# Attention, a routed mixture of experts and an MLP on one core: scores by quarters of the array, and a batch's keys side by side

## What is computed

```python
def _attn_ref(q, k, v, n_sink, window):          # q, k, v: 4 x 8 x 768 x 64, n_sink 4, window 128
    scores = scale * np.matmul(q, k.transpose(0, 1, 3, 2))
    pos = np.arange(S)
    is_sink = pos[None, :] < int(n_sink)
    rel = pos[:, None] - pos[None, :]
    in_window = (rel >= 0) & (rel < int(window))
    keep = is_sink | in_window
    scores = np.where(keep, scores, -1000000000.0)
    scores = scores - np.max(scores, axis=-1, keepdims=True)
    a = np.exp(scores)
    a = a / (np.sum(a, axis=-1, keepdims=True) + 1e-09)
    return np.matmul(a, v).astype(np.float32)
...
    x = np.ascontiguousarray(attn_out.transpose(0, 2, 1, 3)).reshape(B * S, H * D)   # 3072 x 512
    x = _moe_ref(x=x, **moe_kwargs)      # top 1 of 8 experts, 512 -> 1024 -> 512, relu, times the gate
    return _moe2_ref(x=x, **moe2_kwargs) # (h - tanh(h)) @ w_out with h = x @ w_in, 512 -> 2048 -> 512
```

## Time and profile before

| | us |
|---|---|
| runs of the kernel before, median of 3 | 1074.44 (1074.23 to 1078.64) |
| the profiled execution | 1071.83 |
| its span | 1070.1 |
| PE busy over the span | 1058.0 (99%) |
| DVE, ACT, POOL busy | 651.6, 474.8, 504.2 |

### The profile page before, as it was taken

The page is one execution under the profiler, slowest core; times in us unless marked ns, Lnnn a source line. Parts: engine busy times, 40 slices in busy tenths (PEclk is TensorE's granted clock), DMA queues, the critical chain, the costliest instruction groups (busy, mean ns, idle before and its releaser), DMA issues.

```text
span 1070.1 us, 17027 instructions
## 1 busy us (share of the span) xinstructions
PE 1058.0 (99%) x5919; PEld 866.1 (81%) x5919; DVE 651.6 (61%) x1393; ACT 474.8 (44%) x1013; POOL 504.2 (47%) x522
## 2 busy tenths in 40 slices
PE   9999999999999999999999999999999999999997
PEld 6777777888888888888888888888888888888885
DVE  7898895343343434443498666766666666676664
ACT  7988885242143333441644333333333333333332
POOL 4575674661070725770654453444335335344532
PEclk9999999999999999999999999999999999999999
DMA  9647634543142516462411110100101011000001
GB/s 309 205 140 249 215 129 144 197 132 125 51 168 90 197 56 213 169 221 64 140 50 60 51 40 0 42 17 23 30 11 40 11 31 40 1 1 21 20 1 40
DMA packets 38491, 100.16 MB, mean 94 GB/s; under 512 B 8464, under 2 KB 9104, under 8 KB 33296
## 3 DMA queue, kind: packets, MB, share of 16 engines
q1 hardware_dynamic: 29680, 52.68, 15.7%
q0 software_dynamic: 8448, 46.27, 12.2%
q10 hardware_dynamic: 288, 0.26, 0.1%
HBM read 76.06 MB, written 23.13 MB: 93 GB/s over the span
## 4 chain that ended last, share of the span: by engine, by line
PE 91%; DVE 5%; issue 2%; DMA 1%; POOL 1%; ACT 0%; POOLq 0%; DVEq 0%
PE bank L875 24%; PE bank L883 24%; PE bank L818 14%; PE bank L804 14%; PE bank L527 3%; PE bank L565 2%; PE bank L810 2%; PE bank L542 2%; DVE prob L1188 2%; PE bank L791 1%; DVE probT L1204 1%; DMA sorted_x<-x_tok,dest 1%; PE bank L859 1%; PE bank L687 1%; PE bank L589 0%
## 5 line engine op out<-in xcount | busy, mean ns | idle before, releaser
L1673 POOL TENSOR_TENSOR weights<-raw,weights 128x1024 fp32r<-128x1024 f32 x70 | 166.6, 2399 | 187.3 <-ACT weights L943 178.0
L883 PE MATMUL bank<-weights,gT_hi 128*128 128x512 f32 x768 | 238.7, 392 | 0.2 <-DVE gT_lo L1539 0.2
L1796 POOL TENSOR_SCALAR ser<-ser 128x512 f32<-128x512 f32 x96 | 61.6, 642 | 281.0 <-DVE ser L1484 280.9
L875 PE MATMUL bank<-mT_hi,weights 128*128 128x512 f32 x768 | 189.8, 389 | 0.7 <-ACT mT_hi L1112 0.7
L875 PEld LDWEIGHTS bank<-mT_hi,weights 128*128 128x128 f32 x768 | 144.1, 188 | 30.8 <-ACT mT_hi L1112 0.9
L883 PEld LDWEIGHTS bank<-weights,gT_hi 128*128 128x128 f32 x768 | 142.6, 188 | 29.4 <-DVE gT_lo L1539 0.7
L883 PE MATMUL bank<-weights,gT_lo 128*128 128x512 f32 x384 | 149.7, 390 | 0.0
L1126 ACT ACTIVATE bank<-bank 128x512 f32<-128x512 f32 x96 | 55.9, 582 | 210.1 <-DVE ser L1515 210.1
L818 PE MATMUL bank<-weights,hT_hi 128*128 128x512 f32 x448 | 143.5, 401 | 0.0
L804 PE MATMUL bank<-weights,mT_hi 128*128 128x512 f32 x448 | 140.8, 395 | 0.0
L1798 POOL TENSOR_SCALAR sq<-sq 128x512 f32<-128x512 f32 x94 | 140.5, 1495 | 0.0
(11 more groups left out here) (188 smaller groups left out, 1581.8 us busy)
## 6 DMA issues: line engine op xcount, KB each, us to landing
raw<-w_all POOLq DMA_DIRECT2D x32, 1024.0 KB, 5.4
raw<-w_all SPq DMA_DIRECT2D x8, 1024.0 KB, 7.2
sorted_y<-ys SPq DMA_DIRECT2D x30, 261.0 KB, 3.1
xs<-sorted_x SPq DMA_DIRECT2D x29, 261.0 KB, 2.8
v_in<-vt SPq DMA_DIRECT2D x24, 256.0 KB, 3.7
kT<-kt SPq DMA_DIRECT2D x23, 264.0 KB, 3.8
qT<-qt SPq DMA_DIRECT2D x23, 256.0 KB, 4.5
raw<-sorted_y SPq DMA_DIRECT2D x20, 261.0 KB, 2.6
```

What stands on the lines that cost most here:

```text
L875: done = e.matmul(bank[HB[n % 3]][:, :], wt[:, f // 2, c, cols], x[:, c, :], start=(m == 0), stop=(m == 3 * CH - 1))
L883: done = e.matmul(bank[YB[i]][:, :], x[:, n % 3, rows], wt[:, f, :], start=(f == 0 and m == 0), stop=(f == GCH - 1 and m == 2))
L1673: e.tensor_tensor(lo, src, hi.bitcast(F32), ALU.subtract).then_inc(s_w_lo, 1)
L1796: e.tensor_scalar(row, row, SERIES_2, 1.0, ALU.mult, ALU.add).then_inc(s_ser, 1)
```

## The change

Three things, which hang together.

Keys: the ring holds six tiles (a batch), side by side for each pair of heads: 128 keys, 4 sinks, 128 keys, 4 sinks and so on. From the tile before to the own tile one reads 128 + 4 + 128 = 260 columns without a step (`COLS`), the sinks between them. A load of keys now writes four pieces of 528 bytes into a partition instead of one of 2112. One mask serves all tiles with t > 1, one t = 1, and t = 0 has 128 columns, its sinks being among its own keys.

Scores: for t > 0 each head's matmul becomes two of 64 tokens: tokens 0 to 63 meet columns 0 to 195, tokens 64 to 127 meet columns 64 to 259. With two heads that is one matmul in each quarter of the array. What is not written of a bank is masked.

Tiles with t = 1 are treated like those with t > 1 (their sinks are the same keys as some of the tile before; a mask sorts them), and tiles 22 and 23 are merged in all pairs. With that ACT's `part` is gone, and every tile's transposes take the two pairs of a bank together.

```diff
-    COLS = 2 * HALF
+    HP = P // 2
+
+    SINKS, OWN, COLS = P, HALF, HALF + P
...
-    RING_Q, RING_K, RING_V, RING_X = 3, 4, 5, 2 * TILES
+    RING_Q, RING_K, RING_V, RING_X = 3, TILES, 5, 2 * TILES
...
-    def is_merged(g, p):
-        return g % TILES > 1 and (p % 2 == 0 or g < ALL - 2)
...
+    sink_tiles = [g for g in range(ALL) if g % TILES]
...
-        kT = sb("kT", [P, RING_K, PAIRS, HALF], F32, keys)
+        kT = sb("kT", [P, PAIRS, RING_K * HALF], F32, keys)
...
+        def keys_of(g, h, first, last):
+
+            at = g % TILES * HALF
+            return kT[D * (h % 2):D * (h % 2) + D, h // 2, at + first:at + last]
...
             def load_keys(g):
-                e.dma_start(kT[:, g % RING_K, :, :].rearrange("p a n -> p (a n)"), kt[g, :, :]).then_inc(k_in[g % RING_K], 16)
+                at = g % RING_K * HALF
+                e.dma_start(kT[:, :, at:at + HALF], kt[g, :, :].rearrange("p (a n) -> p a n", a=PAIRS)).then_inc(k_in[g % RING_K], 16)
...
-                cols = HALF if t == 0 else COLS
-                for h in (2 * pair, 2 * pair + 1):
-                    rows = slice(D * (h % 2), D * (h % 2) + D)
+                heads = (2 * pair, 2 * pair + 1)
+                for h in heads:
                     if H * g + h >= 4:
                         e.wait_ge(s_masked, H * g + h - 3)
-                    e.matmul(bank[S_BANK[h % 4]][:, 0:cols].rearrange("p (n c) -> p n c", c=HALF),
-                             qT[rows, g % RING_Q, pair, :], keys_of(g, h), start=True, stop=True).then_inc(s_scores, 1)
...
+                for n in range(2):
+                    for h in heads:
+                        done = e.matmul(bank[S_BANK[h % 4]][n * HP:(n + 1) * HP, n * HP:COLS - HP + n * HP],
+                                        qT[D * (h % 2):D * (h % 2) + D, g % RING_Q, pair, n * HP:(n + 1) * HP],
+                                        keys_of(g - 1, h, n * HP, COLS - HP + n * HP), start=True, stop=True,
+                                        skip_group_check=True)
+                        if n:
+                            done.then_inc(s_scores, 1)
...
-                sinks = in_values and g % TILES > 1
+                sinks = in_values and g in sink_count
...
-                if not in_one_bank(i):
-                    turn_prob(i, (1,))
 
             logits(ALL - 2)
-            turn_prob(ALL - 1, (2,))
-            early_up(0, range(2, 4))
-            turn_prob(ALL - 1, (3,))
-            early_up(0, range(4, 6))
+            early_up(0, range(2, 6))
+            turn_prob(ALL - 1, (2, 3))
...
-                if part_on_act(i, 1):
-                    part(i, 1)
...
-                    if i < ALL and is_merged(i, p):
+                    if i in sink_count:
                         merge(i, p)
```

More of the change, by code:

```diff
@@ L536, in turn_prob @@
                         e.wait_ge(s_exp, H * g + 2 * p + 2)
-                    halves = (0, 1) if not is_merged(g, p) and t else (0,)
                     for n in range(2):
-                        for side in halves:
-                            half = 1 - side if len(halves) == 2 and own_first(g) else side
-                            at = 2 * P * k + (len(halves) * n + side) * P
-                            done = e.transpose(bk[:, at:at + P], prob[:, g % 2, 2 * p + n, half, 0:P], ident[:, :])
+                        at = 2 * P * k + n * P
+                        done = e.transpose(bk[:, at:at + P], prob[:, g % 2, 2 * p + n, OWN:COLS], ident[:, :])
                 done.then_inc(s_turned, len(pairs))
@@ L1014, in scalar @@
                     exp(i, h)
-                if g >= 0 and part_on_act(g, 3):
-                    part(g, 3)
-                if g >= 0 and g % TILES > 1:
+                if g in sink_count:
                     sinks_evict(g)
@@ L1036, in scalar @@
             logits_evict(ALL - 2)
-            part(ALL - 1, 3)
             sinks_evict(ALL - 1)
@@ L1342, in vector @@
                     if h == 3 and g >= 0:
-                        for p in (2, 3):
-                            if not part_on_act(g, p):
-                                part(g, p)
+                        part(g, 2)
+                        part(g, 3)
                 at_once(routing)
@@ L1357, in vector @@
                     add_logits(w)
-                if not part_on_act(i, 1):
-                    part(i, 1)
+                part(i, 1)
                 if i % TILES == 1:
@@ L1365, in vector @@
             part(ALL - 1, 2)
+            part(ALL - 1, 3)
             at_once(ranks_read)
@@ L1589, in gpsimd @@
         def gpsimd(e):
-            own = {order: mask[:, order, 1 - order, 0:P] for order in range(2)}
-            prev = {order: mask[:, order, order, 0:P] for order in range(2)}
             step = [0]
@@ L1621, in gpsimd @@
-            seen_by_next(e.tensor_copy(mask_t1[:, :, :], mask[:, 0, :, :]))
-            e.memset(mask_t1[:, 0, 0:n_sink], 0.0)
-            e.memset(mask_t1[:, 0, P:HALF], FILL).then_inc(c_masks, 1)
-            e.wait_ge(c_zero, 2)
+                    seen_by_next(op)
+                    op = e.affine_select(out=part, in_=part, compare_op=ALU.is_gt, fill=FILL, base=window,
+                                         pattern=[[1, P]], channel_multiplier=-1)
+                return op
+            seen_by_next(own_keys(mask_t0[:, :]))
```

172 lines of the change are left out of this document (59 added, 113 removed).

## The result

The changed kernel took **1081.09 us** (median, 1079.08 to 1084.24) where the kernel before took 1074.99 beside it (1074.11 to 1078.64). The ratio is **1.0055, interval 1.0039 to 1.0071**: slower by some 6 us. I had forecast 1075.0 and a range up to 1079.5, so both the number and the range were wrong. Run again in two later groups, the ratio was 1.0037 (1.0026 to 1.0049) and 1.0036 (1.0022 to 1.0051). So the loss is 4 to 6 us.

What follows compares the result with a forecast made beforehand. PE bounds only some tiles of the first 182 us; DVE, ACT and POOL hold the rest. Terms -2.55 + 0.3 + 2.3 + 0.1 + 0.4 = +0.55 us on 1074.44 gave 1075.0, range 1070.0 to 1079.5.

Steps and rivals of the forecast that it cites:

- quarters, tiles 3, 4, 10, 11, 16, 17: PE-bound tiles: narrower score blocks save 1.0 in tiles 3 and 4, 1.0 in 10 and 16, 0.6 in 11 and 17.
- tiles 1 and 2: Start of the first batch: merges hold tile 1 up by 0.5 us, score blocks give 0.6 back: -0.1.
- tiles 5 to 7: ACT is full there, so quarters save 0; tile 7's merges take the place of a shed eviction: +0.15 us.
- tile 8: DVE, busy 6.34 of 6.61 us, gets an added multiply of 0.6, of which some 0.3 fits idle time: +0.3.
- tiles 12 to 14, 18 to 20: Merges wait behind POOL's scatters: first mask +0.57, one more part in tile 14 +0.6, together +1.15 us, twice: +2.3.
- last tiles: Tiles 22 and 23: POOL's waits and gaps absorb 2.85 us of merges, last scatter stays at 173.1 to 173.2: +0.1.
- start: First loads: PE waits for tile 1's queries behind two loads of keys in short pieces: +0.4 us (0 to 1.2).
- rivals 1 and 2: Score blocks: first, quarters' loads do not overlap, 1077.7 us, chance 0.08; second, only two quarters run at once, 1088, 0.10.
- the third group, DVE-bound: Tiles with t = 3 in batches 1 to 3 (9, 15, 21): DVE sets the period, so the quarters save 0.
- two blocks a tile, 0.5 us: Scores: each four-head block saves 0.25 us, two blocks a tile, reaching the end only where PE sets the period.
- DVE has room: Tiles with t = 1: one added DVE multiply, 0.6 us in a row of them, fits into that period.
- My slower rival: Score blocks: only two quarters run at once, 0.43 us more a block, 1088 us in all, chance 0.10.

Runs made afterwards that it cites:

- quiet profiles: Profiles from groups of runs in which the kernel before took 1071.1 to 1071.2 us; for the changed kernel, an execution of 1075.55 us.
- e8: Changed kernel with two tiles' keys in one load from tile 2 on (pieces of 1056 bytes); ratio 1.0039 to the kernel before.
- e7: Kernel before with its keys stored pair by pair in DRAM, so that loads come in 528-byte pieces; ratio 1.0000.
- e12: Changed kernel with all new merges undone (t = 1, and pairs 1 and 3 of the last two tiles); 1071.07 us, ratio 0.9991.
- e14: Changed kernel with all new merges undone, and in t = 1 the sinks and the quarters too; ratio 1.0001 to the kernel before.
- c1_before: Kernel before, unchanged, profiled again as a control in a group where it took 1074 us and up; ratio 1.0002.
- e13: Changed kernel with POOL's sink cast and token numbers moved behind the merges of pairs 0 and 1; ratio 1.0034 to the kernel before.
- e3: Changed kernel with the merges of pairs 1 and 3 of tiles 22 and 23 undone; 1079.16 us, ratio 1.0044.
- late profile: Profile from a group of runs in which the kernel before took 1074 us and up.
- e16: Changed kernel with merges undone for pairs 1 and 3 only, in t = 1 and in the last two tiles; ratio 1.0038.

## Why the prediction was wrong, point by point

By the quiet profiles, tile by tile (periods of the changed kernel less those of before):

| term | forecast | measured |
|---|---|---|
| quarters, tiles 3, 4, 10, 11, 16, 17 | -2.6 | -0.8 |
| tiles 1 and 2 | -0.1 | +0.85 |
| tiles 5 to 7 | +0.15 | +0.3 |
| tile 8 | +0.3 | +0.3 |
| tiles 12 to 14, 18 to 20 | +1.15 each | +0.6, +0.65 |
| last tiles | +0.1 | +0.7 |
| start | +0.4 | -0.1 (+1.7 in the first profile) |
| sum | +0.55 (with tiles 9, 15, 21 at 0) | +2.4 |

The profile has 1.7 us more in tile 2 (8.28 us, 6.62 in the other runs), where its clock was halved from 16.34 to 19.75; that makes 4.06. The medians of the quiet groups differ by 4.2 to 4.6, and e8's profile, with no such stretch, only by 2.5 from that of before. Those two are not typical executions: the profiled one of before took 0.7 more than its quiet median, e8's 1.3 less than its own. Where the slower executions of e8 lose their 1.3 is open.

- **Right:** a block at 0.82 (0.84 to 0.86 forecast), so rivals 1 and 2 are refuted; the path through tile 13 (forecast: the first mask behind it late by 1.2; measured 1.3, and 0.8 behind tile 19); the third group, DVE-bound, unmoved; e7 for the keys. On the loads, an item of the Trainium skill ("TensorE: Matmul & The Clock Gate", packing small matmuls) has them overlap only where the row group differs. The trace still does not agree: 16 records of quarters take 0.82 us, although the quarters of one head share their rows.
- **Right by luck:** the +0.3 of tile 8. I had put it down to DVE's added part, but e12, without the merges, has the tile at 7.21, longer still, and e14, without the sinks of t = 1 too, at 6.62. And the +0.3 of tiles 5 to 7 is tile 6 shorter by 0.4 and tile 7 longer by 0.75.
- **The step that failed, "two blocks a tile, 0.5 us":** only the first block got shorter. The second had 1.30 in the chain of the kernel before, where the first had 1.09. Those 0.21 us were the sign that it was already waiting, for masks: four banks of scores hold one block, and in the kernel before DVE's four masks of tile 4 last from 26.77 to 28.33. The end of the fourth is this row, and the first weight load for the block's last head starts at 28.39, right behind it:

```profile
28.25 0.08 DVE L1188 DVE_READ_ACCUMULATOR2_ANT negmax<- 128x1 f32 x1
```

  A saving on a block that waits is none. From the 6.82 of 6.82 busy I had concluded that PE sets the period; matmuls that overlap their own waits look busy. The failure is worth 1.8 us.
- **The merges were mis-sized in the easy places.** In t = 1 I had written that "DVE has room". It has, but not at that point: part 1 and the sinks' remainder run back to back in front of the next tile's first mask. Chain of waits in tile 1 of the quiet profile:

```profile
12.59 0.68 DVE probT L1147
13.27 0.03 issue
13.30 0.75 DVE v_sink L1156
14.05 0.03 issue
14.08 0.04 DVE prob L1137
```

  The 0.68 is the added part, and tile 1 is longer by 0.65; tile 7 by 0.75. In the dear places I had too much (1.15 each, not 0.65). That the longer tile 13 takes over what tile 14 had waited for (6.90 instead of 7.50) I had in the sum; the +0.6 for one more part in tile 14 is what did not come. In the profile read for the kernel before, DVE waited 0.57 us there for a scatter to land, and 0.40 in tile 20. In c1_before both waits are absent and tile 14 takes 6.85, so that the part came to 0.05; against its 19.43 and 19.49 the quiet changed kernel loses 1.2 and 1.1. What the change costs in these places thus varies with the execution of before that it is held against.
- **The last tiles: that POOL's gaps would take the 2.85 us of merges was wrong.** Ahead of the scatter at 166.67 POOL had waited for DVE's destinations; ahead of that at 171.00 it still does (1.19 instead of 1.79), and DVE is what is late. From tile 23 to the last scatter it is 18.90 us, where it was 17.34, and PE idles 2.0 us there instead of standing busy. POOL and SP in the quiet profile:

```profile
171.00 0.99 POOL L1648 DMA_INDIRECT sorted_x<-x_tok,dest  x1 [1.19 <-DVE dest L1239]
...
177.41 0.96 POOL L1648 DMA_INDIRECT sorted_x<-x_tok,dest  x1 [0.30 <-issue]
```
```profile
181.75 0.37 SPq L370 DMA_DIRECT2D xs<-sorted_x  x1
```

  Why DVE is late I had nowhere in the sum, neither its two added parts a tile nor this: two of its small routing instructions, each with two inputs from SBUF, are held while POOL merges: `seen`, here in the quiet profile with the two merges beside it and then before, and `shift`, 0.75 instead of 0.18. Together they take 1.5 us more; 0.2 comes back at `hot_all`, which a merge had held in the kernel before (0.52 instead of 0.75).

```profile
165.03 1.12 DVE L1222 TENSOR_TENSOR seen<-seen,key 128x8 f32<-128x8 f32 x1
164.70 1.42 POOL L1592 TENSOR_TENSOR prob<-prob 128x256 f32<-128x256 f32 x2
```
```profile
161.15 0.22 DVE L1277 TENSOR_TENSOR seen<-seen,key 128x8 f32<-128x8 f32 x1
```

  All five profiles of e8, e13 and the changed kernel have `seen` at 1.12 there, and e3 and e12, without the added merges of the last tiles, at 0.21. How the 1.56 us to the last scatter divide between the parts and the hold no run separates. I had priced such a hold only as a bound, for another instruction.
- **The range** left out what the clock does with such gaps. Two of the places where PE idles more now, tiles 1 and 2 and the last tiles, stand in front of a halved clock in some execution (from 16.34 in one of the changed kernel's three profiles, from 175.94 and 177.34 in the other two); the gaps of 0.95 us in tile 13 do not, and the kernel before has such a stretch too, from 172.36 in its late profile. I had priced idle time at its own length. My slower rival was the wrong one: the loss needed no fault of the quarters.

## What to carry to other kernels

When a block of work shows longer in the chain of waits than its sister of the same size, the difference is a wait, and shortening the block gives nothing: price a saving by the shortest instance. A part moved to an engine "with room" is priced by what stands right behind it in that engine's order, not by the engine's idle share. A change that trades work of the bounding engine for waits between the others should be undone piece by piece: here the quarters gain 1.6 to 1.8 us beside the same kernel without them, the merges that came with them lose 4.4, and with the merges undone nothing beyond the measurement is left over the kernel before. And a new instruction on one engine can lengthen those of another without any semaphore between them: compare the durations of the small instructions beside it, not only the waits.

## What the runs showed of the hardware

**A collision worth 4.4 us.** In the first profile of the changed kernel the expert stages took 892.4 us behind the join instead of 888.0. DVE's scaling of the next slot's rows and POOL's weight split, both with two inputs from SBUF, in that profile; then the DVE row of the changed kernel in the other late group:

```profile
475.59 5.15 DVE L1374 TENSOR_TENSOR xs<-xs 128x512 f32<-128x512 f32 x1 [4.10 <-DMA xs<-sorted_x]
```
```profile
475.47 4.71 POOL L1621 TENSOR_TENSOR weights<-raw,weights 128x1024 fp32r<-128x1024 f32 x2
```
```profile
472.95 1.70 DVE L1374 TENSOR_TENSOR xs<-xs 128x512 f32<-128x512 f32 x1 [1.97 <-DMA xs<-sorted_x]
```

The slot's rows landed 0.1 us after POOL had begun, and DVE, whose median for this instruction is 0.69, was held until both of POOL's instructions were done. PE then idled 2.65 us and ran 3.41 us at half clock. In the profiles of e14 and e16 the instruction takes 5.57 and 5.26, PE idles 2.8 us from 473.2 and 475.4, and 892.7 and 892.5 us lie behind the join. To be held behind one of POOL's is common: the kernel before has this instruction at 3.1 to 3.2 us six times, the one at 464 us among them, and PE has no idle stretch over 0.7 us anywhere behind them in the expert stages. The Trainium skill ("SBUF — State Buffer", two separate sides) calls the port that the two share an exclusive lock for a whole instruction. The trace agrees, and shows it kept over two of POOL's in a row, here as in `seen` above (165.03 to 166.15, POOL's two merges until 166.12).

**Matmuls whose semaphores come microseconds after their records** (the "remote" waits) appear in whole groups of runs, in both kernels, and go with about 3 us more in the kernel before (1074 against 1071 us). Their cause is open.
